# Gated attention and two expert layers on one core: separate tiles for the second unit's gates, and a reciprocal by logarithm and exponential

## The reference

```python
mag = np.sqrt(a_re * a_re + a_im * a_im)
scale = np.minimum(mag, 0.999) / (mag + 1e-06)
a_re_n, a_im_n = a_re * scale, a_im * scale
for t in range(S):          # per batch and head; state S_re, S_im is 48 x 48
    S_re, S_im = ar * S_re - ai * S_im + outer(k[t], v[t]), ar * S_im + ai * S_re
    y[t] = q[t] @ S_re
```

## Time and profile before

| what | us |
|---|---|
| median of 3 runs (972.25 to 975.63) | 973.26 |
| the profiled execution | 980.33 |
| its span | 978.6 |
| PE busy | 858.2 (88%) |
| DVE busy | 567.6 (58%) |
| ACT busy | 416.4 (43%) |
| POOL busy | 372.6 (38%) |

### The profile page before, as it was taken

How to read it: one execution, slowest core, us unless ns; L and a number is a source line. 1 busy time by engine, 2 the same in 40 slices (tenths; PEclk the granted TensorE clock), 3 DMA queues, 4 the chain that set the end, 5 groups by cost and what they waited for, 6 DMA issues and landing times.

```text
span 978.6 us, 14428 instructions
## 1 busy us (share of the span) xinstructions
PE 858.2 (88%) x5692; PEld 742.6 (76%) x5692; DVE 567.6 (58%) x738; ACT 416.4 (43%) x589; POOL 372.6 (38%) x273
## 2 busy tenths in 40 slices
PE   0152688898999999989999989999999999999997
PEld 0152687887887788778877768887898989898987
DVE  5477998786979797979797852354312121212120
ACT  4446574636474746464656532443212121212121
POOL 3036364453545353545363522353613131313110
PEclk9966798988999999999999999999999999999999
DMA  8421525253424343444334243303010100000000
GB/s 340 120 75 49 164 66 164 83 151 111 136 85 130 117 131 94 122 132 115 100 115 137 77 136 116 140 1 113 1 44 23 39 27 34 32 33 0 31 3 33
DMA packets 70724, 88.46 MB, mean 90 GB/s; under 512 B 15360, under 2 KB 55296, under 8 KB 70144
## 3 DMA queue, kind: packets, MB, share of 16 engines
q1 hardware_dynamic: 70656, 87.53, 29.0%
HBM read 59.13 MB, written 28.39 MB: 89 GB/s over the span
## 4 chain that ended last, share of the span: by engine, by line
PE 43%; DVE 27%; issue 14%; ACT 7%; DMA 4%; POOL 3%; SPq 0%; DVEq 0%; POOLq 0%; ACTq 0%
PE bank L1061 43%; DVE t L807 3%; DVE t L826 3%; DVE ge L801 3%; DVE st L807 3%; DVE t L804 2%; DVE t L853 2%; DMA qt<-q_cols 2%; DVE kp L807 2%; DVE ge L804 2%; DVE qp L807 1%; DVE t L869 1%; DVE t L801 1%; DVE sc L807 1%; ACT t L594 1%
## 5 line engine op out<-in xcount | busy, mean ns | idle before, releaser
L482 POOL TENSOR_TENSOR gl<-ge,gh 128x512 fp32r<-128x512 f32 x96 | 133.3, 1388 | 228.2 <-ACT gh L594 227.3
L807 DVE TENSOR_TENSOR hm<-bank,hm 128x512 f32<-128x512 f32 x72 | 49.8, 692 | 226.5 <-PE bank L1061 224.7
L1061 PE MATMUL bank<-xh,wih 128*128 128x512 f32 (+1 forms) x336 | 127.8, 380 | 26.0 <-DVE xl L807 24.9
L1061 PE MATMUL bank<-gh,woh 128*128 128x512 f32 (+1 forms) x336 | 126.3, 376 | 5.9 <-ACT x2s L594 5.2
L1061 PE MATMUL bank<-xh,wal 128*128 128x512 f32 x324 | 126.1, 389 | 0.0
L1061 PE MATMUL bank<-xl,wah 128*128 128x512 f32 x324 | 126.1, 389 | 0.0
L1061 PE MATMUL bank<-xh,wah 128*128 128x512 f32 x324 | 126.0, 389 | 0.0
L482 POOL TENSOR_TENSOR hl<-hm,hh 128x512 fp32r<-128x512 f32 x36 | 46.5, 1293 | 205.8 <-ACT hh L594 205.8
L1061 PE MATMUL bank<-xl,wih 128*128 128x512 f32 (+1 forms) x336 | 123.5, 368 | 0.0
L1061 PE MATMUL bank<-xh,wil 128*128 128x512 f32 (+1 forms) x336 | 123.4, 367 | 0.0
L1061 PE MATMUL bank<-gl,woh 128*128 128x512 f32 (+1 forms) x336 | 121.9, 363 | 0.0
(11 more groups left out here) (89 smaller groups left out, 1744.4 us busy)
## 6 DMA issues: line engine op xcount, KB each, us to landing
q_cols<-qp SPq DMA_DIRECT2D x24, 384.0 KB, 2.8
qt<-q_cols SPq DMA_DIRECT2D x24, 384.0 KB, 4.1
k_cols<-kp SPq DMA_DIRECT2D x24, 384.0 KB, 3.0
kt<-k_cols SPq DMA_DIRECT2D x24, 384.0 KB, 4.3
vv<-in_v SPq DMA_DIRECT2D x12, 448.0 KB, 5.1
ar<-in_a_re SPq DMA_DIRECT2D x12, 384.0 KB, 3.2
ai<-in_a_im SPq DMA_DIRECT2D x12, 384.0 KB, 4.5
kd<-in_k SPq DMA_DIRECT2D x12, 384.0 KB, 6.6
```

What stands on the lines that cost most here:

```text
L482: return nc.gpsimd.tensor_tensor(dst, whole, high.bitcast(f32), ALU.subtract)
L807: return nc.vector.tensor_tensor(dst, a, b, op)
L1061: return nc.tensor.matmul(dst, lhsT, rhs, start=start, stop=stop)
```

## The change

Unit 1 gets its own tiles for the gates, q and k (`ar2` ... `cs2`), at addresses of tiles that are in use only later: in the upper halves of `wih` and `woh` and in `xh`. The later writers of these places get waits. `gates(u)` names a unit's set, `users(u)` how many earlier users of this set there were. The loads get two semaphores in turn. The reciprocal of the denominator becomes Ln and Exp with scale -1 on ACT (`inverse`). For that the denominator is made positive: |ar| + mag, with |ar| by Abs on ACT in the square root's table, and the sign moves behind the arctangent (`signed`), where angles are counted in quarters of a turn. Square root and arctangent stay with their tables. The weights' loads go from two calls of two parts, in front of all, to four of one part at `w_load`. All three position tables are written anew.

```diff
 AT (offsets of units 2 to 11; those that changed most)
-        "reciprocal_a": -15, "reciprocal_b": -12, "negative": -11, "decayed_a": -7, "decayed_b": -8,
+        "inverse": -15, "signed": -8, "negative": -17, "decayed_a": -10, "decayed_b": -7,
-        "rotate_q_a": -3, "rotate_k_a": -2, "rotate_q_b": 2, "rotate_k_b": 4, "s_a": 4, "store_q_b": 4, "store_k_b": 4,
+        "rotate_q_a": -4, "rotate_k_a": -2, "rotate_q_b": 3, "rotate_k_b": 6, "s_a": 5, "store_q_b": 6, "store_k_b": 7,
 AT_FIRST (unit 0)
-        "square": -17, "root": -17, "denominator": -14, "scan_lam": -14, "exps": -10, "sines": -5, "rotate_k_b": -1,
+        "square": -28, "root": -25, "denominator": -26, "scan_lam": -19, "exps": -16, "sines": -12, "rotate_k_b": -11,
 AT_SECOND (unit 1; position 16 + offset)
-        "square": -13, "root": -12, "scan_lam": -9, "exps": -8, "sines": -3, "rotate_q_a": -3, "rotate_k_b": 3,
+        "square": -36, "root": -34, "scan_lam": -31, "exps": -26, "sines": -25, "rotate_q_a": -23, "rotate_k_b": -17,
-        "load_a": -17, "load_q": -11, "load_k": -13, "load_qt_a": -3, "s_a": 2,
+        "load_a": -42, "load_q": -42, "load_k": -41, "load_qt_a": -8, "s_a": 4,
 SPLIT
-        "w_in_high": (-1, 0, 16, 19), "w_out_high": (5, 9, 12, 24), "w_in_low": (6, 13, 18, 23), "w_out_low": (3, 9, 15, 30),
+        "w_in_high": (-2, 7, 18, 21), "w_out_high": (2, 10, 11, 26), "w_in_low": (11, 12, 18, 23), "w_out_low": (2, 3, 15, 28),
+        "w_load": (-15, -8, 0, 8),
...
+        usual = Gates(*(t[:, :, :] for t in (ar, ai, qd, kd, t1, t2, t3, sn, cs)))
+        second = Gates(*(t[:, :, :] for t in (ar2, ai2, qd2, kd2, t12, t22, t32, sn2, cs2)))
+        def gates(u):
+            return second if u == 1 else usual
+        def users(u):
+            return 0 if u < 2 else 1 if u == 2 else u
...
             def load_a(u):
-                if u >= 1:
-                    sp.wait_ge(phi0, u)
-                sp.dma_start(ar[:, :, :], unit(a_re, u)).then_inc(l_a, 16)
+                if users(u):
+                    sp.wait_ge(phi0, users(u))
+                sp.dma_start(gates(u).ar, unit(a_re, u)).then_inc(l_a[u % 2], 16)
...
             def root(u):
                 nc.scalar.preload_act_table(ACT.Sqrt)
...
-                func(t1[:, :, :], t2[:, :, :], ACT.Sqrt).then_inc(mag, 1)
+                func(g.t1, g.t2, ACT.Sqrt).then_inc(mag, 1)
+                func(g.t3, g.ar, ACT.Abs).then_inc(mag, 1)
                 back()
             def ln_first(u):
-                act.wait_ge(sgn, u + 1)
+                act.wait_ge(den, u + 1)
...
+            def inverse(u):
+                g = gates(u)
+                act.wait_ge(den, u + 1)
+                func(g.t2, g.t2, ACT.Ln).then_inc(lnd, 1)
+                act.wait_ge(lnd, u + 1)
+                func(g.t2, g.t2, ACT.Exp, scale=-1.0).then_inc(inv, 1)
...
             def x_high(n):
+                if n == B:
+                    act.wait_ge(rr, UPC)
             def w_in_high(z):
+                if z == 2:
+                    act.wait_ge(tan, UPC)
+                    act.wait_ge(phi0, UPC)
+                if z == 3:
+                    act.wait_ge(qpd, UPC * PAIR)
+                    act.wait_ge(kpd, UPC * PAIR)
             def w_out_high(z):
+                if z == 2:
+                    act.wait_ge(trig, 2 * UPC)
+                    act.wait_ge(rr, UPC)
+                if z == 3:
+                    act.wait_ge(qpd, UPC * PAIR)
+                    act.wait_ge(kpd, UPC * PAIR)
...
             def squared(u):
                 stt(t2[:, :, :], t3[:, :, :], M2_LEAST, t2[:, :, :], ALU.max, ALU.add).then_inc(m2, 1)
-                dve.wait_ge(m2, u + 1)
-                ts(t3[:, :, :], ar[:, :, :], 0.0, ALU.is_lt, -2.0, ALU.mult).then_inc(neg, 1)
             def denominator(u):
-                stt(t2[:, :, :], t3[:, :, :], 1.0, t1[:, :, :], ALU.add, ALU.mult).then_inc(sgn, 1)
-                dve.wait_ge(sgn, u + 1)
-                tt(t2[:, :, :], ar[:, :, :], t2[:, :, :], ALU.add).then_inc(den, 1)
-            def reciprocal(u, e):
-                dve.wait_ge(den, u + 1)
-                nc.vector.reciprocal(t2[:, e, :], t2[:, e, :]).then_inc(rec, 1)
+                dve.wait_ge(mag, 2 * u + 2)
+                tt(g.t2, g.t3, g.t1, ALU.add).then_inc(den, 1)
             def negative(u):
-                ts(ar[:, :, :], ar[:, :, :], 0.0, ALU.is_lt, 0.5, ALU.mult).then_inc(neg2, 1)
+                ts(g.ar, g.ar, 0.0, ALU.is_lt, -2.0, ALU.mult).then_inc(neg, 1)
+            def signed(u):
+                stt(g.t2, g.ar, 1.0, g.t2, ALU.add, ALU.mult).then_inc(sgn, 1)
             def angle(u):
-                stt(t2[:, :, :], t2[:, :, :], 1.0 / math.pi, ar[:, :, :], ALU.mult, ALU.add).then_inc(phi0, 1)
+                stt(g.t2, g.t2, -4.0 / math.pi, g.ar, ALU.mult, ALU.add).then_inc(phi0, 1)
```

More of the change, by code:

```diff
@@ L1 @@
 import math
+from collections import namedtuple
 from contextlib import ExitStack
@@ L59, in build @@
-        "s_a": 4, "s_b": 10, "kr_a": 5, "kr_b": 11, "masked_a": 4, "masked_b": 10, "kr_evac_a": 6, "kr_evac_b": 11,
-        "state_decayed_a": 4, "state_decayed_b": 6, "y_a": 6, "y_b": 11, "inc_a": 9, "inc_b": 13, "state_add_a": 9,
-        "state_add_b": 14, "x_high_a": 6, "x_low_a": 8, "x_high_b": 12, "x_low_b": 12, "load_a": -22, "load_q": -8,
-        "load_k": -8, "load_v": 3, "store_q_a": -4, "load_qt_a": -2, "store_k_a": -3, "load_kt_a": 0, "store_q_b": 4,
-        "load_qt_b": 5, "store_k_b": 4, "load_kt_b": 9, "store_ends": -5, "load_ends": -5, "tile": 13,
+        "inverse": -15, "clamp": -17, "log_decay": -15, "signed": -8, "tangent": -11, "arctan": -9, "angle": -8,
@@ new lines, in build @@
+        "scan_lam": -10, "center": -10, "exps": -7, "ends": -7, "scan_phi": -7, "reduced": -6, "decayed_a": -10,
+        "decayed_b": -7, "sines": -4, "rotate_q_a": -4, "rotate_k_a": -2, "rotate_q_b": 3, "rotate_k_b": 6, "state_decay": 2,
+        "s_a": 5, "s_b": 10, "kr_a": 6, "kr_b": 11, "masked_a": 5, "masked_b": 10, "kr_evac_a": 5, "kr_evac_b": 11,
+        "state_decayed_a": 5, "state_decayed_b": 7, "y_a": 7, "y_b": 11, "inc_a": 9, "inc_b": 13, "state_add_a": 9,
+        "state_add_b": 14, "x_high_a": 7, "x_low_a": 8, "x_high_b": 12, "x_low_b": 12, "load_a": -22, "load_q": -7,
@@ L64, in build @@
+        "load_k": -8, "load_v": 4, "store_q_a": -4, "load_qt_a": -2, "store_k_a": -3, "load_kt_a": -1, "store_q_b": 6,
+        "load_qt_b": 7, "store_k_b": 7, "load_kt_b": 9, "store_ends": -5, "load_ends": -4, "tile": 13, "negative": -17,
     }
     AT_FIRST = {
-        "square": -17, "square_im": -20, "squared": -17, "root": -17, "denominator": -14, "ln_first": -16, "ln_second": -13,
-        "reciprocal_a": -10, "clamp": -14, "log_decay": -18, "reciprocal_b": -11, "negative": -11, "tangent": -10, "arctan": -9,
@@ L74, in build @@
-        "load_q": -17, "load_k": -22, "load_v": -11, "store_q_a": -8, "load_qt_a": -7, "store_k_a": -7, "load_kt_a": -3,
-        "store_q_b": -4, "load_qt_b": -1, "store_k_b": -3, "load_kt_b": -3, "store_ends": -1, "load_ends": 2, "tile": 11,
+        "square": -28, "square_im": -32, "squared": -26, "root": -25, "denominator": -26, "ln_first": -25, "ln_second": -21,
+        "inverse": -21, "clamp": -22, "log_decay": -21, "signed": -18, "tangent": -21, "arctan": -19, "angle": -17,
+        "scan_lam": -19, "center": -18, "exps": -16, "ends": -16, "scan_phi": -15, "reduced": -13, "decayed_a": -16,
@@ L76, in build @@
+        "store_q_b": -10, "load_qt_b": -9, "store_k_b": -9, "load_kt_b": -7, "store_ends": -17, "load_ends": -11, "tile": 8,
+        "negative": -21,
     }
     AT_SECOND = {
-        "square": -13, "square_im": -13, "squared": -16, "root": -12, "denominator": -13, "ln_first": -12, "ln_second": -12,
-        "reciprocal_a": -9, "clamp": -11, "log_decay": -13, "reciprocal_b": -6, "negative": -11, "tangent": -8, "arctan": -6,
-        "angle": -6, "scan_lam": -9, "center": -8, "exps": -8, "ends": -6, "scan_phi": -6, "reduced": -6, "decayed_a": -7,
@@ L87, in build @@
-        "load_qt_b": 7, "store_k_b": 7, "load_kt_b": 8, "store_ends": -10, "load_ends": -6, "tile": 15,
+        "square": -36, "square_im": -37, "squared": -39, "root": -34, "denominator": -34, "ln_first": -34, "ln_second": -34,
+        "inverse": -33, "clamp": -33, "log_decay": -33, "signed": -30, "tangent": -32, "arctan": -29, "angle": -28,
+        "scan_lam": -31, "center": -30, "exps": -26, "ends": -26, "scan_phi": -25, "reduced": -25, "decayed_a": -24,
+        "decayed_b": -24, "sines": -25, "rotate_q_a": -23, "rotate_k_a": -20, "rotate_q_b": -18, "rotate_k_b": -17,
@@ L88, in build @@
+        "negative": -34,
     }
@@ L733, in attention @@
                     ln_second(at(x, "ln_second"))
+                if now("inverse"):
+                    inverse(at(x, "inverse"))
                 if now("arctan"):
@@ L1011, in attention @@
                     negative(at(x, "negative"))
+                if now("signed"):
```

(1 more changed line is left out.)

223 lines of the change are left out of this document (125 added, 98 removed).

## The result

| kernel | median us | runs | ratio to before (95% interval) |
|---|---|---|---|
| before | 973.93 | 4 | 1 |
| changed | 980.63 | 4 | 1.0068 [1.0046, 1.0090] |

Slower by 0.7%, where 943.4 us was forecast and 964 was the upper end. The changed kernel's profiled execution took 981.53 us (span 979.8), that of before 980.33 (span 978.6). The two traces therefore show only 1.2 us of the 6.7 us between the medians, because the profiled execution of before was a long one of its kind (980.33 where its median is 973.93). Where in the kernel the other 5.5 us lie, no trace shows. What follows compares stretches of the traces, and sizes of effects on the whole time are taken from ratios.

What follows compares the result with a forecast made beforehand. PE was taken as the bound from 226.2 us on, with 98.4 of 120.4 idle us before that. Gains 7.6 + 5.3 + 14 + 3 = 29.9 off the 973.26 us median gave 943.4 us, range 924 to 964.

Steps and rivals of the forecast that it cites:

- later chunks: Stretch from 226.2 us on: freer DVE shortens mask and `xl` waits by 6, Abs and inverse cost 3; gain 3 us.
- groups 3 to 16: Middle of attention: 13.1 us of column and `xl` waits and 6 of low clock mostly go; gain 14 us.
- first group: Start: first `xh` x `wih` matmul at 79.5 us instead of 87.15, unit 0's mask at 59.7; gain 7.6 us.
- first three groups: From first to fourth group: the 12.49 us column wait goes, waits of 5.5 and 4.3 come; gain 5.3 us.
- the rest: Part of 19 us in the attention's middle not taken as gain: waits for masks and `xl` that stay.
- Rival B: Column waits of 5.6 and 4.5 us before units 2's and 3's scores return; 958 us, chance 0.17.
- D: ACT's queue between expert exponentials becomes the bound, 4.05 us lost in each of ten units; 981 us, chance 0.08.
- the sign named for D: A period of two units above 95.5 us in the middle would show ACT's queue as the bound.
- B's sign: More than 10 us idle before scores of units 2 and 3 would show that column waits stay.
- E: Start not faster: unit 0 pays 7.6 us more, first groups stall 5.3 on weights' low parts; 956 us, chance 0.09.
- the prediction's rule against it: Before the first group, DVE and POOL block each other: six meetings of 1 us, making the gain 24, 949 us.

Runs made afterwards that it cites:

- second trace: The changed kernel run again unedited, compared with the kernel before: 981.71 us, ratio 1.0052.

## Why the prediction was wrong, point by point

The forecast of 29.9 us missed the traces' 1.2 us lost by 31.1: 10.2 in the later chunks, 11.6 in groups 3 to 16, 5.1 at the first group and 4.2 in the first three groups. So two thirds of the miss lie in the start, and the later chunks turned what was left of the gain into a loss.

**Later chunks (forecast gain 3, came out 7.2 lost, 4.8 in the second trace): this step decided the sign.** It counted what ACT gets more of and what DVE gets less of, and charged Abs on PE's path at the exponential of the earlier trace rows. That place did not show. The wait grew at the token-tile boundary, at the copies of `x2s`, of which I had the total in the earlier trace rows (5.2 us) and asked nothing about what stands ahead of them in DVE's queue. The diff gives the answer: the sign test, in the old table behind the reciprocals at -11, goes to -17, where the boundary's copy follows it. Moving that one number back gives 1.6%, moving the copies instead gives 1.5%. Of the 4.07 us lost from one boundary to the next, 2.2 are the longer wait and most of the rest the slow matmuls behind it.

**Groups 3 to 16 (forecast 14, came out 2.4).** The step took 13.1 us of waits as gone. The column waits did go, 5.62 and 4.47 to 1.40 and 0.83, with a new one of 0.98, and the scores behind them took 2.02 us instead of 3.75. But `xl` still waits 1.28 us, and four mask waits came, 2.63, 1.16, 1.20 and 2.29 us, which the step had put at "the rest". PE's idle time from the fourth group on is 13.8 us instead of 16.7. And its busy time did not fall by the 6 us taken for the clock, it is 91.2 instead of 90.8 at granted clock 0.95: the stretch now begins with the eighteen matmuls of the fourth group 0.21 us apart, where before they were 0.12 apart. Rival B feared the columns and D the exponential; neither feared the second mask. The one experiment on it showed that these waits are a trade: mask earlier, columns late.

**First group (forecast 7.6, came out 2.5).** Unit 0's mask came at 69.84, not 59.7. The rotations and mask were in the order foreseen, but the store that unit 1's third rotation waits for landed late: 6.87 us of waiting where 2.8 were taken from the median of the earlier trace rows. That median is taken mostly from the middle. Here the weights' loads of 768 KB are in flight, and early weights halve it. This and the store before it explain 6.6 of the 10.1 us. The other 3.5 were there before unit 1's first rotation (56.85, forecast 53.3), and they fit POOL's meetings with DVE, shown below. The rest of the path, from mask to group, was 14.8 us, where 19.8 had been taken, so half of the error was hidden by luck. (The step's own addition gives 79.3, not 79.5. And DVE's 82 us for two units, in proportion of the fourth stage, are 79.6. Neither matters to the result.)

**First three groups (forecast 5.3, came out 1.1).** The first group was 2.5 us early and the fourth 3.6. The wait of 7.24 us for the first elu was foreseen at 5.5: ACT's timeline has unit 2's square, which waited for the load of `ai`, and the root block ahead of group 0's exponential:

```profile
88.58 0.85 ACT L633 ACTIVATE t<-ar 128x768 f32<-128x768 f32 x1 [5.19 <-DMA ai<-in_a_im]
...
90.82 1.28 ACT L647 ACT_TABLE_LOAD   x1
...
98.54 0.58 ACT L633 ACTIVATE ge<-bank 128x512 f32<-128x512 f32 x1
```

So the chain was the one named, behind a load, and the mask wait after it was 2.67 us instead of 4.3. The sum missed in the step's own terms: waits of 5.5 and 4.3 in place of 12.5 leave 2.7, and the other 2.6 of the 5.3 were given no reason. What came were waits of 1.06, 7.24 (until 101.21, for the elu) and 2.67 (until 110.70, for the mask), 1.5 less than the 12.49 of before, and 1.1 us were gained. The Ln at 97.79 stood on DVE's denominator, and that behind a low part of `w_in` of 4.99 us, beside POOL's low part of `w_out` of 3.57.

**The rivals.** D's 981 us is the measured time, by luck: it comes from 4.05 us lost in each of ten units and the whole gain in front. D had the sign and half of the place. ACT is busier by 26 us and the period did pass 95.5, the sign named for D, but the middle lost 4 us in two units, at the token-tile boundary, and the larger part goes with one instruction on DVE. Taking Abs out gives 1.0%, moving the sign test 1.6%, and both act at one and the same wait. B's sign (over 10 us idle before the scores of units 2 and 3) stayed away: 1.40 and 0.83. E was right that the start gains little; I had given it 0.09. Its reason, POOL and DVE meeting, did show. DVE in the changed kernel, then POOL:

```profile
19.66 1.76 DVE L921 TENSOR_TENSOR_SCAN t<-restart,t 128x768 f32<-128x768 f32 x1 [1.69 <-POOL t L514]
...
28.19 3.34 DVE L921 TENSOR_TENSOR_SCAN t<-restart,t 128x768 f32<-128x768 f32 x1 [1.70 <-POOL t L514]
...
35.45 0.96 DVE L928 COPY ends<-t 128x12 f32<-128x12 f32 x1
...
91.07 4.99 DVE L875 TENSOR_TENSOR wil<-wir,wih 128x1536 fp32r<-128x1536 f32 x1
```

```profile
28.11 1.80 POOL L514 TENSOR_TENSOR t<-ai,t 128x768 f32<-128x768 f32 x1
...
90.88 3.57 POOL L517 TENSOR_TENSOR wol<-wor,woh 128x1536 fp32r<-128x1536 f32 x1 [0.79 <-ACT woh L633]
```

POOL works without a pause from 25.70 to 37.33 and from 45.37 to 50.37. Seven DVE instructions beside it, from the scan at 28.19 to the rotation at 49.44, took 6.2 us more than the same ones in this trace without POOL beside them (1.76 for the scan at 19.66, 0.17 for the copy at 23.52). That is the six us of the prediction's rule against it, which the sum had left out; with the low part of `w_in` at 91.07 (2.22 us at 78.19) it is more. The late store behind the weights comes on top.

**The rule in the middle.** The sign test took 0.55 us at 17.42 in the changed kernel and 1.64 us at 333.60. DVE in the start, then POOL beside the second of them, then the sign test's group in the kernel before:

```profile
17.42 0.55 DVE L869 TENSOR_SCALAR ar<-ar 128x768 f32<-128x768 f32 x1
```

```profile
333.56 1.26 POOL L517 TENSOR_TENSOR gl<-ge,gh 128x512 fp32r<-128x512 f32 x1 [5.36 <-ACT gh L633]
```

```profile
L801 DVE TENSOR_SCALAR ar<-ar 128x768 f32<-128x768 f32 x12 | 14.0, 1169 | 0.0
```

The Trainium skill, SBUF — State Buffer, section "Who interferes with whom", says that a DVE tensor_scalar in its two-port form and a GpSimd instruction shut each other out for a whole instruction. The trace agrees: POOL's low part began at 333.56, 0.04 us before the sign test, which took 1.1 us more than at 17.42. I had used that rule for the start alone. In the middle it makes a 0.55 us instruction ahead of the copy one of 1.64 us. The row of the kernel before already had it at 1.17 us in the mean of twelve; I had priced only the other sign test, at 0.89. The elu's own tensor_scalar rose the same way, from 540 to 713 ns in the mean over 96, 16.5 us in all, which is most of the 23 us that DVE's fall in busy time is short of the forecast. Of the 88 elu steps that the timeline lists, 26 took over 0.6 us, and each of these has a POOL instruction beside it.

**What stays open.** Why the changed kernel's two traces differ in their stages (periods of 99.6, 99.5, 99.1 and of 96.8, 98.8, 98.6) with equal spans. Where the 5.5 us lie that the medians show beyond the two profiled executions. What the sign test would cost in its place without POOL beside it; no run has that. And the mask wait of 11 us in front of the fourth group, in the two kernels with unit 2 later: no order tried removes it.

## What to carry to other kernels

When work is moved in a queue, look first at the rare instructions behind it, such as the copy that frees a bank once per tile. A busy share shows nothing of them, and one short instruction ahead of such a copy cost most of its length on PE here (1.4 of 1.64 us), and often more through the clock. Count each stall of a start together with the one that is next in line: two that hide each other gave the first group 0.2 and 0.9 us alone and 7.5 together. Trace the same kernel twice before a difference of 2 or 3 us in one stage is given a cause. Take the duration of a store from rows of the stage in which it stands, not from the median over the run.

## What the runs showed of the hardware

The lower clock behind a wait is not a function of the wait's length. These are all waits of PE for `x2s` amid full load, in the fourteen traces, with the number of matmuls 0.43 us apart that followed:

| wait, us | cases | slow matmuls behind it |
|---|---|---|
| 1.35 to 1.61 | 3 | none |
| 1.87 to 2.22 | 17 | none in 10, eight in 7 |
| 2.84 to 2.88 | 12 | none in 2, seven or eight in 10 |
| 3.04 to 4.31 | 21 | seven to fourteen in all |

Eight such matmuls cost 1.6 us on top of the wait. In the same kernel one wait of 1.87 us cost nothing more and the next but one, of 1.88, cost 1.6. I had priced low clock only in the start.

A fp32 tensor_scalar of 128x768 on DVE took 0.55 us in the start and 1.64 to 1.68 in units 4 to 11, each time beside a POOL instruction that had begun before it; with the sign test one group later its longest was 2.12 us. Where DVE's began first, as at 17.42 with POOL's at 17.57, it took 0.55.
